# Gate logits in six tiles of 128 tokens, finished inside the down product, with x sums, GpSimd's weight work and the first Sinkhorn hops at other places

## The chip, the cores and the metric

The kernel runs on one NeuronCore of a Trainium2 chip. The metric is device time in microseconds of one execution; lower is better. PE is TensorE, DVE is VectorE, ACT is ScalarE, POOL is GpSimd, SP is the queue that issues the transfers.

## What is computed

Sliding-window attention (4 batches, 8 heads, 576 positions, 64 wide, window 64) feeds a dense layer with an ELU, and that feeds a layer of eight experts whose output is weighted by a gate. The gate is what the change touches.

```python
def _moe_ref(x, w_in, w_out):                 # x 2304 x 512, d_ff 2048
    h = x @ w_in
    g = np.where(h > 0.0, h, alpha * (np.exp(np.minimum(h, 0.0)) - 1.0))
    return (g @ w_out)

def _moe2_ref(x, w_gate, w1, w2):             # 8 experts, F 1024
    logits = x @ w_gate
    logits = logits - logits.max()
    P = np.exp(logits)
    for _ in range(8):
        P /= P.sum(1, keepdims=True) + 1e-09
        P /= P.sum(0, keepdims=True) + 1e-09
        P *= N / E
    for e in range(E):
        h = np.maximum(x @ w1[e], 0.0)
        ye = h @ w2[e]
        out += P[:, e:e + 1] * ye
```

## The kernel before

After the attention the program goes through 60 rounds: 20 groups of 512 hidden columns (4 of the dense layer, 16 of the experts), each for 3 chunks of 768 tokens. The block products are done with seven products in place of eight (a Strassen form), so a round has seven up products (`ps<-xs,w1t`) and seven down products (`ps<-ss,w2t`). Each product is 12 matmuls of 128 x 384: three for each of four operand pairs, since every operand is a high and a low part (`hi`, `lo`). The kernel's loop goes by windows w: window w does the up steps of round w and the down steps of round w-1 in turn, up 0, down 0, up 1, down 1, to step 6. I write up (w,s) for the up product of step s in window w, and down (w,s) for the down product that follows it in the same window.

All five engines run hand-written orders and are joined by counting semaphores; there is no scheduler. In each window ACT copies products out of PSUM (`snap_*`, L710) and makes the high parts (`hi`, L763); DVE adds products (`add_c`, L970), adds the down products to the sum `yacc` (`add_y`, L1044), makes low parts (`lo`, L942), the activation (`act_f`, L1017; `relu` on ACT, L788, for some rounds) and the Strassen sums s1 to s4 (L949 to L965); POOL splits weights (`weight_sum_*`, `weight_lo`, L542 to L565). A semaphore counts each: `c_done` up products, `d_done` down products, `c_read` the `add_c`, `s_lo_done` the `lo`, `y_read` and `y_copied` the `add_y` of a step. `wait_f(engine, r, 4)` waits until the fourth activation of round r is there; up (w,1) needs it of round w-1.

Windows 11 to 13 (`GATE_WINDOW` to before `MAX_WINDOW`) have extra work. The dense layer's result of chunk c is ready in `yacc` then, and DVE and ACT turn it into the experts' operand: four sums of quarters (`x_sum`, L984 to L998, places in the table `XSUMS`) and seven high and low parts (`x_hi` L683, `x_lo` L905, places in `XPREP`), which up products of window 12 and later read directly. In the same windows PE makes the gate's logits in `hop`, which `product` calls in the middle of an up product, after 7 of its 12 matmuls:

- steps 1, 2 and 3: two token tiles each, a matmul for every quarter of the 512 columns of x, the four into four groups of 32 partitions (L1339);
- a step later ACT has put these parts into `logit_parts` (`move_parts`, L718), and PE adds the four groups up with the constant `adder` (L1331), transposed, into free columns of the up product's banks; ACT (L721) or DVE (L1091) moves eight logits for each token to `gate`;
- the last two of the eight tiles of 96 tokens are done at step 1 the other way round, with `yacc` as the weights and eight moving columns (L1348).

From window 14 come the eight Sinkhorn steps: DVE normalises rows and sums columns over tiles (`rows_then_parts`), PE sums over partitions (a hop, L1361), DVE normalises columns (`columns`). The list `SINK_HOPS` says at which up product each hop stands. After the eighth the table is turned and stored, and window 18 is the first that uses it.

Of the kernel before, what the change touches and what calls it, by code (L numbers as in the profile page):

```python
# [12 lines left out]
P = 128  # L13
# [14 lines left out]
def build_program(nc, q, k, v, w_in, w_out, w_gate, w1, w2, out):  # L28
# [39 lines left out]
    TT = 96  # L68
# [14 lines left out]
    for w, cc in [(1, 2)] + [(GATE_WINDOW + c, CHUNKS + c) for c in range(CHUNKS)]:  # L83
# [5 lines left out]
        XSUMS[0 if cc < CHUNKS else w][0 if cc < CHUNKS else 3] = [(cc, 0), (cc, 1)]  # L89
# [34 lines left out]
    SINK_HOPS = [(MAX_WINDOW, 3), (MAX_WINDOW, 5)]  # L124
# [4 lines left out]
    with ExitStack() as ctx:  # L129
# [25 lines left out]
        p_turned = logit_parts[0:TT]  # L155
# [82 lines left out]
        def hop_spare(w, step):  # L238
            return spare(w, step, 0, HT + TT + 4 * step, HT + TT + 4 * step + E)[0:TT, :]

        def c_spare(r, step, a, b):
            s = (r + step) % 2
            return ps[:, 2 * s:2 * s + 2, a:b]

# [77 lines left out]
        stored = sem("stored")  # L322

# [77 lines left out]
        def _(sp):  # L401
# [70 lines left out]
            for w in range(ROUNDS):  # L472
                g, c = divmod(w, CHUNKS)
                e, half = divmod(g - FF_GROUPS, HALVES)
                for step in range(STEPS):
# [8 lines left out]
                    if w == SCALE_WINDOW - 1 and step == 1:  # L484
                        for i in range(2):
                            sp.wait_ge(p_placed, 1)
                            sp.dma_start(p_store[i * TT:(i + 1) * TT, :], p_turned[:, i, :]).then_inc(p_stored, 16)
# [24 lines left out]
        def _(pool):  # L512
# [88 lines left out]
            for w in range(ROUNDS):  # L601
# [18 lines left out]
                if w >= 1:  # L620
                    pool.wait_ge(s_lo_done, STEPS * (w - 1) + STEPS)
# [25 lines left out]
        def _(act):  # L647
# [64 lines left out]
            def tiles(w, first):  # L712

                t = (w - GATE_WINDOW) * CHUNK_TILES + first
                return gate[:, :, t:t + 2].rearrange("p e t -> p t e")

            def move_parts(w, step):
                nc.scalar.activation(logit_parts[:], c_spare(w, step, HT, HT + TT), ACT.Copy).then_inc(parts_placed, 1)  # L718

            def move_logits(w, step, first, at):  # L720
                nc.scalar.activation(tiles(w, first), c_spare(w, step, HT + at, HT + at + E)[0:TT], ACT.Copy) \  # L721
                    .then_inc(logits_moved, 1)

            def gate_work(w, step):
# [3 lines left out]
                if step == 1:  # L728
                    move_logits(w, step, CHUNK_TILES - 2, TT + E)
                else:  # L730
                    move_logits(w, step, 2 * (step - 2), TT)
                move_parts(w, step)
# [75 lines left out]
            for w in range(ROUNDS + 1):  # L808
# [49 lines left out]
                gate_work(w, 1)  # L858
# [3 lines left out]
                gate_work(w, 2)  # L862
# [6 lines left out]
                gate_work(w, 3)  # L869
# [20 lines left out]
        def _(dve):  # L890
# [177 lines left out]
            def columns(k):  # L1068
# [6 lines left out]
                elif step == 5:  # L1075
                    dve.wait_ge(c_done, STEPS * w + step + 1)
                nc.vector.tensor_scalar(col_norm[0:TT], hop_spare(w, step), EPS, None, ALU.add).then_inc(col_read, 1)
# [10 lines left out]
            def gate_work(w, at):  # L1088
                if at == 4 and GATE_WINDOW <= w < MAX_WINDOW:
                    t = (w - GATE_WINDOW) * CHUNK_TILES + 4  # L1090
                    nc.vector.tensor_copy(gate[:, :, t:t + 2].rearrange("p e t -> p t e"),  # L1091
                                          c_spare(w, 4, HT + TT + E, HT + TT + 2 * E)[0:TT]).then_inc(logits_placed, 1)
                if w == MAX_WINDOW - 1 and at == 4:
                    dve.wait_ge(logits_placed, CHUNKS)
                    dve.wait_ge(logits_moved, 3 * CHUNKS)
                    nc.vector.tensor_reduce(token_max[0:TT], gate[:], AX.XY, ALU.max).then_inc(token_maxed, 1)
                if w == MAX_WINDOW - 1 and at == 5:
                    dve.wait_ge(max_turned, 1)
                    dve.wait_ge(c_done, STEPS * w + 6)
                    nc.vector.tensor_reduce(all_max[:], spare(w, 5, 0, HT, HT + TT)[0:1, :], AX.X, ALU.max,  # L1100
                                            negate=True).then_inc(all_maxed, 1)
                if w == MAX_WINDOW and at == 0:
# [3 lines left out]
                    nc.vector.tensor_copy(gate_shift[0:TT], spare(w, 0, 0, HT + TT, HT + TT + 1)[0:TT, :]) \  # L1106
# [11 lines left out]
                if (w, at) == P_HOP:  # L1118
# [3 lines left out]
                    nc.vector.tensor_copy(p_turned, c_spare(w, at, HT, HT + TT)[0:TT]).then_inc(p_placed, 1)  # L1122

            def x_piece(w, at):
                for cc, i in XSUMS[w][at]:
                    x_sum(cc, i)
# [302 lines left out]
```

## Time and profile before

| | |
|---|---|
| time, median of 3 runs | 1929.63 us (1926.22 to 1929.71) |
| the profiled execution | 1927.98 us, of which its span 1926.1 us |
| busy share of the span | PE 98%, DVE 79%, ACT 44%, POOL 34% |
| chain that ended last | PE 90%, DVE 5% |
| three kinds of large matmul of up and down, 1680 each | 10080, mean 336 to 339 ns, overlapped in pairs |

A busy PE is not a PE at its peak, since matmuls overlap. A timeline's first column is the start in us from the span's start, the second the length; the distance from one start to the next is what an instruction costs on PE. In brackets stands how long the engine idled before it and what released it.

### The profile page before, as it was taken

What the parts mean: (1) busy time and instruction counts of PE and PEld (TensorE: products, weight loads), DVE (VectorE), ACT (ScalarE), POOL (GpSimd) and SP (SyncE); (2) the same over time, 40 slices, a digit from 0 to 9 for tenths busy, and PEclk for the clock granted to TensorE, in tenths of its full rate; (3) what the DMA queues carried; (4) which work ended last, traced back from release to release, by engine and by line L of the source; (5) the groups of instructions that cost most, each with busy time, mean ns of one, the idle gap of its engine ahead of it and who ended that gap; (6) DMA issues with size and microseconds to landing.
All of it is one profiled execution on the core that took longest, in us unless ns stands there. A gap on an engine that the chain in (4) does not pass through costs nothing.

```text
span 1926.1 us, 31391 instructions
## 1 busy us (share of the span) xinstructions
PE 1883.2 (98%) x11676; PEld 1847.0 (96%) x11676; DVE 1526.8 (79%) x1840; ACT 853.1 (44%) x1419; POOL 651.9 (34%) x512
## 2 busy tenths in 40 slices
PE   8889999999999999999999999999999999999998
PEld 6669999998889999999999999999999999999998
DVE  6987878777889888787787787787787787877877
ACT  7767656555556443343333342332433332433422
POOL 5643332332232434332423324233323233233220
PEclk9999999999999999999999999999999999999999
DMA  9974766663357666666566666666666666666654
GB/s 250 278 283 143 250 215 206 216 207 134 152 194 243 237 223 215 222 225 235 200 241 213 217 213 226 212 216 227 218 231 207 229 221 211 219 227 210 212 187 148
DMA packets 96710, 414.75 MB, mean 215 GB/s; under 512 B 9776, under 2 KB 10800, under 8 KB 96560
## 3 DMA queue, kind: packets, MB, share of 16 engines
q1 hardware_dynamic: 96560, 412.74, 63.0%
q8 instruction: 95, 1.56, 0.3%
q14 instruction: 55, 0.45, 0.1%
HBM read 374.88 MB, written 37.82 MB: 214 GB/s over the span
## 4 chain that ended last, share of the span: by engine, by line
PE 90%; DVE 5%; issue 2%; ACT 1%; POOL 1%; DMA 1%; DVEq 0%; SPq 0%; ACTq 0%; POOLq 0%
PE ps L1269 29%; PE ps L1264 29%; PE ps L1271 29%; PE ps L1228 1%; PE ps L1254 1%; DMA scratch<-v_dram 1%; PE ps L1244 1%; DVE hb L1017 1%; DVE xs L905 0%; DVE hb L970 0%; DVE ss L942 0%; DVE scratch L919 0%; ACT pb L775 0%; POOL scratch L536 0%; DVE yacc L1044 0%
## 5 line engine op out<-in xcount | busy, mean ns | idle before, releaser
L763 ACT ACTIVATE ss<-hb 128x768 fp32r<-128x768 f32 x420 | 347.8, 843 | 602.1 <-DVE hb L1024 281.4
L1264 PE MATMUL ps<-xs,w1t 128*128 128x384 f32 x1680 | 569.0, 339 | 8.9 <-DVE hb L1017 4.1
L1269 PE MATMUL ps<-xs,w1t 128*128 128x384 f32 x1680 | 569.5, 339 | 0.0
L1264 PE MATMUL ps<-ss,w2t 128*128 128x384 f32 x1680 | 564.5, 336 | 2.5 <-DVE yacc L1044 2.5
L1271 PE MATMUL ps<-ss,w2t 128*128 128x384 f32 x1680 | 566.1, 337 | 0.0
L1271 PE MATMUL ps<-xs,w1t 128*128 128x384 f32 x1680 | 566.0, 337 | 0.0
L1269 PE MATMUL ps<-ss,w2t 128*128 128x384 f32 x1680 | 563.9, 336 | 0.0
L1044 DVE TENSOR_TENSOR yacc<-ps,yacc 128x768 f32<-128x768 f32 x396 | 377.9, 954 | 176.8 <-PE ps L1271 171.7
L942 DVE TENSOR_TENSOR ss<-hb,ss 128x768 fp32r<-128x768 f32 x420 | 400.0, 956 | 21.8 <-ACT ss L763 11.5
L565 POOL TENSOR_TENSOR w1t<-wraw,w1t 128x512 fp32r<-128x512 f32 x140 | 187.3, 1350 | 511.9 <-DVE ss L942 327.4
L565 POOL TENSOR_TENSOR w2t<-wraw,w2t 128x512 fp32r<-128x512 f32 x140 | 183.7, 1330 | 427.0 <-DVE hb L965 229.0
L1264 PEld LDWEIGHTS ps<-xs,w1t 128*128 128x128 f32 x1680 | 315.8, 188 | 11.1 <-issue 6.7
L1264 PEld LDWEIGHTS ps<-ss,w2t 128*128 128x128 f32 x1680 | 316.8, 189 | 3.7 <-DVE ss L942 2.5
L1269 PEld LDWEIGHTS ps<-xs,w1t 128*128 128x128 f32 x1680 | 316.8, 189 | 1.1 <-issue 0.2
L1271 PEld LDWEIGHTS ps<-xs,w1t 128*128 128x128 f32 x1680 | 316.6, 188 | 0.0
L1271 PEld LDWEIGHTS ps<-ss,w2t 128*128 128x128 f32 x1680 | 316.5, 188 | 0.0
L1269 PEld LDWEIGHTS ps<-ss,w2t 128*128 128x128 f32 x1680 | 316.5, 188 | 0.0
L970 DVE TENSOR_TENSOR hb<-ps,hb 128x768 f32<-128x768 f32 x180 | 172.1, 956 | 138.6 <-PE ps L1271 138.1
L710 ACT ACTIVATE hb<-ps 128x768 f32<-128x768 f32 x180 | 145.2, 807 | 156.7 <-PE ps L1271 155.7
L1024 DVE SCALAR_TENSOR_TENSOR hb<-hb,pb 128x768 f32<-128x768 f32 x126 | 130.6, 1036 | 2.9
L660 ACT ACTIVATE w2t<-wraw 128x512 fp32r<-128x512 f32 x140 | 87.1, 622 | 89.5 <-PE ps L1271 89.5
L542 POOL TENSOR_TENSOR wraw<-wraw 128x512 f32<-128x512 f32 x40 | 53.1, 1328 | 194.0 <-DVE hb L965 194.0
(100 smaller groups left out, 1342.6 us busy)
## 6 DMA issues: line engine op xcount, KB each, us to landing
xs<-x_store SPq DMA_DIRECT2D x388, 768.0 KB, 4.3
wraw<-moe_w_dram SPq DMA_DIRECT2D x32, 1024.0 KB, 7.0
x_store<-xs SPq DMA_DIRECT2D x32, 768.0 KB, 4.1
pb<-p_store SPq DMA_DIRECT2D x24, 384.0 KB, 4.0
x_store<-w2t SPq DMA_DIRECT2D x10, 768.0 KB, 3.9
scratch<-q_dram SPq DMA_DIRECT2D x16, 288.0 KB, 4.9
scratch<-k_dram SPq DMA_DIRECT2D x16, 288.0 KB, 7.5
scratch<-v_dram SPq DMA_DIRECT2D x16, 288.0 KB, 7.8
```

Source lines behind the costliest of these rows:

```text
L542: nc.gpsimd.tensor_tensor(wtmp[i][:, 0], w_quarter(i, 0, 1), w_quarter(i, 0, 0), ALU.subtract) \
L565: nc.gpsimd.tensor_tensor(pair2(wt[i][:, step, 1, :]), w_operand(i, step), pair2(wt[i][:, step, 0, :].bitcast(F32)), ALU.subtract) \
L660: nc.scalar.activation(pair2(wt[i][:, step, 0, :]), w_operand(i, step), ACT.Copy) \
L710: nc.scalar.activation(pair2(hq(r, quarter)), c_banks(r, step), ACT.Copy).then_inc(c_snap, 1)
L763: nc.scalar.activation(ss[:, step, 0, :], hq(r, HOME[step]), ACT.Copy).then_inc(s_hi_done, 1)
L942: nc.vector.tensor_tensor(ss[:, step, 1, :], hq(r, HOME[step]), ss[:, step, 0, :].bitcast(F32), ALU.subtract).then_inc(s_lo_done, 1)
L970: nc.vector.tensor_tensor(pair2(hq(r, quarter)), c_banks(r, step), pair2(hq(r, quarter)), ALU.add) \
L1024: nc.vector.scalar_tensor_tensor(h, src, 0.0, weight, ALU.max, ALU.mult).then_inc(f_done, 1)
L1044: nc.vector.tensor_tensor(acc, d_banks(r, step), acc, ALU.add).then_inc(y_read, 1)
L1264: nc.tensor.matmul(bank, w_parts[:, step, 0, cols], hi, start=step in FRESH and kt == 0, stop=False, skip_group_check=True)
L1269: nc.tensor.matmul(bank, w_parts[:, step, 0, cols], lo, start=False, stop=False, skip_group_check=True)
L1271: last = nc.tensor.matmul(bank, w_parts[:, step, 1, cols], hi, start=False, stop=kt == 1, skip_group_check=True)
```

## The change

The tiles are 128 tokens, so six instead of eight for each chunk and 18 in all. All six are made by quarters (steps 1, 2 and 3, tiles 4-5, 0-1 and 2-3), and the `yacc`-as-weights form is gone. The adding up stands one product later, in the middle of down step 2, 3 or 4, in the free columns of the down product's bank (`d_spare`). `move_parts` at steps 2 and 3 now waits for that step's down product too. All logits of a chunk are moved by two copies instead of four. Hop 1 no longer waits for the last add to `yacc` (step 6 of round w-2), only for step 5; hop 2 waits for step 6. On DVE the first two x sums go from place 3 to place 2 of the window, ahead of `add_y` of step 3. POOL's third batch of weight work in windows 11 to 13 waits for `add_c` of step 4 instead of a low part that is long there. The first two Sinkhorn hops go from window 14's steps 3 and 5 to steps 4 and 6, DVE's parts of them with them. The turn of the maxima goes into down step 5.

```diff
-    TT = 96
+    TT = P
-        XSUMS[0 if cc < CHUNKS else w][0 if cc < CHUNKS else 3] = [(cc, 0), (cc, 1)]
+        XSUMS[0 if cc < CHUNKS else w][0 if cc < CHUNKS else 2] = [(cc, 0), (cc, 1)]
-    SINK_HOPS = [(MAX_WINDOW, 3), (MAX_WINDOW, 5)]
+    SINK_HOPS = [(MAX_WINDOW, 4), (MAX_WINDOW, 6)]
...
+        GATE_TILES = {1: 4, 2: 0, 3: 2}
...
-                if w >= 1:
+                if GATE_WINDOW <= w < MAX_WINDOW:
+                    pool.wait_ge(c_read, 3 * w + 2)
+                elif w >= 1:
                     pool.wait_ge(s_lo_done, STEPS * (w - 1) + STEPS)
...
             def move_parts(w, step):
-                nc.scalar.activation(logit_parts[:], c_spare(w, step, HT, HT + TT), ACT.Copy).then_inc(parts_placed, 1)
-            def move_logits(w, step, first, at):
-                nc.scalar.activation(tiles(w, first), c_spare(w, step, HT + at, HT + at + E)[0:TT], ACT.Copy) \
-                    .then_inc(logits_moved, 1)
-            def gate_work(w, step):
                 if not GATE_WINDOW <= w < MAX_WINDOW:
                     return
                 act.wait_ge(c_done, STEPS * w + step + 1)
+                if step >= 2:
+                    act.wait_ge(d_done, STEPS * (w - 1) + step + 1)
+                nc.scalar.activation(logit_parts[:], c_spare(w, step, HT, HT + TT), ACT.Copy).then_inc(parts_placed, 1)
...
             def gate_work(w, at):
+                if at == 3 and GATE_WINDOW <= w < MAX_WINDOW - 1:
+                    dve.wait_ge(d_done, STEPS * (w - 1) + 4)
+                    nc.vector.tensor_copy(logits_of(w - GATE_WINDOW, 0, 2), summed(w, 3, 0, 2)).then_inc(logits_placed, 1)
                 if at == 4 and GATE_WINDOW <= w < MAX_WINDOW:
+                    dve.wait_ge(d_done, STEPS * (w - 1) + 5)
+                    nc.vector.tensor_copy(logits_of(w - GATE_WINDOW, 2, CHUNK_TILES), summed(w, 4, 2, CHUNK_TILES)) \
+                        .then_inc(logits_placed, 1)
...
                 x_piece(w, 2)
+                gate_work(w, 3)
                 if down:
                     add_y(before, 3)
...
                 x_piece(w, 3)
-                gate_work(w, 3)
...
-                product(d_banks(r, step), step, w2t, step, ss, d_done)
+                product(d_banks(r, step), step, w2t, step, ss, d_done, between=lambda: down_hop(r + 1, step))
...
                     if step == 1:
-                        wait_y(pe, FF_ROUNDS - CHUNKS + c1, 6)
+                        wait_y(pe, FF_ROUNDS - CHUNKS + c1, 5)
+                    if step == 2:
+                        wait_y(pe, FF_ROUNDS - CHUNKS + c1, 6)
-                    if step >= 2:
-                        pe.wait_ge(parts_placed, 3 * c1 + step - 1)
...
-                    if step == 1:
-                        for j in range(2):
-                            first = c1 * CT + (CHUNK_TILES - 2 + j) * TT
-                            at = HT + TT + E
-                            for kt in range(KT):
-                                nc.tensor.matmul(spare(w, step, j, at, at + E)[0:TT, :], yacc[:, kt, first:first + TT],
-                                                 wg[:, kt, 0:E], start=False, stop=kt == KT - 1, skip_group_check=True)
...
+            def down_hop(w, step):
+                if GATE_WINDOW <= w < MAX_WINDOW and step - 1 in GATE_TILES:
+                    pe.wait_ge(parts_placed, 3 * (w - GATE_WINDOW) + step - 1)
+                    for j in range(2):
+                        t = GATE_TILES[step - 1] + j
+                        nc.tensor.matmul(d_spare(w - 1, step, 0, E * t, E * (t + 1)), logit_parts[:, j, :], adder[:],
+                                         start=False, stop=True, skip_group_check=True)
```

PE's order, in window 11 before, the middle of up step 2 (`xs,w1t` is an up product):

```order
L1264 MATMUL ps<-xs,w1t 128x384
L1331 MATMUL ps<-adder,logit_parts 96x8 x2
L1339 MATMUL ps<-yacc,wg 32x96 x8
L1269 MATMUL ps<-xs,w1t 128x384
L1271 MATMUL ps<-xs,w1t 128x384
```

and now, the same place and on into down step 2 (`ss,w2t`):

```order
L1292 MATMUL ps<-xs,w1t 128x384
L1362 MATMUL ps<-yacc,wg 32x128 x8
L1297 MATMUL ps<-xs,w1t 128x384
...
L1299 MATMUL ps<-ss,w2t 128x384
L1292 MATMUL ps<-ss,w2t 128x384
L1389 MATMUL ps<-adder,logit_parts 128x8 x2
L1297 MATMUL ps<-ss,w2t 128x384
```

The adding up moved from the head of the hop in the up product to the middle of the next product, 12 large matmuls later.

DVE's order in window 12 before, from the low part of step 6 (`ss<-hb,ss`); `yacc<-ps,yacc` is `add_y`, `yacc<-yacc` and `pb<-yacc` are the first two x sums, `hb<-ps,hb` is `add_c` of step 4:

```order
L942 TENSOR_TENSOR ss<-hb,ss 128x768
L905 TENSOR_TENSOR xs<-yacc,xs 128x768
L1044 TENSOR_TENSOR yacc<-ps,yacc 128x2x384
L984 TENSOR_TENSOR yacc<-yacc 128x2x384
L990 TENSOR_TENSOR pb<-yacc 128x768
L905 TENSOR_TENSOR xs<-yacc,xs 128x768 x2
L970 TENSOR_TENSOR hb<-ps,hb 128x768
L1091 COPY gate<-ps 96x2x8
```

and now:

```order
L956 TENSOR_TENSOR ss<-hb,ss 128x768
L919 TENSOR_TENSOR xs<-yacc,xs 128x768
L998 TENSOR_TENSOR yacc<-yacc 128x2x384
L1004 TENSOR_TENSOR pb<-yacc 128x768
L1108 COPY gate<-ps 128x2x8
L1058 TENSOR_TENSOR yacc<-ps,yacc 128x2x384
L919 TENSOR_TENSOR xs<-yacc,xs 128x768 x2
L984 TENSOR_TENSOR hb<-ps,hb 128x768
L1111 COPY gate<-ps 128x4x8
```

The two x sums stand ahead of `add_y` of step 3, with a first small copy of logits between them.

POOL's order in window 11 before, with the semaphores that each instruction waits for; `w1t` is weight_lo, `wraw` a weight sum:

```order
L565 TENSOR_TENSOR w1t<-wraw,w1t 128x512 [waits w_hi_done0,s_lo_done]
L548 TENSOR_TENSOR wraw<-wraw 128x2x256 [waits w_added1]
L565 TENSOR_TENSOR w1t<-wraw,w1t 128x512 [waits w_hi_done0,s_lo_done]
L565 TENSOR_TENSOR w1t<-wraw,w1t 128x512 [waits w_hi_done0]
L552 TENSOR_TENSOR wraw<-wraw 128x512
```

and now:

```order
L580 TENSOR_TENSOR w1t<-wraw,w1t 128x512 [waits w_hi_done0,s_lo_done]
L563 TENSOR_TENSOR wraw<-wraw 128x2x256 [waits w_added1]
L580 TENSOR_TENSOR w1t<-wraw,w1t 128x512 [waits w_hi_done0,c_read]
L580 TENSOR_TENSOR w1t<-wraw,w1t 128x512 [waits w_hi_done0]
L567 TENSOR_TENSOR wraw<-wraw 128x512
```

The last three of these now stand behind DVE's `add_c` of step 4.

## Rows read from the trace of the kernel before

**Rows 1.** Busy time of the engines by stretches: us, then PE, PEld, DVE, ACT, POOL, clock

```profile
437.30:585.00 147.70, 136.97 (x907) 131.28 (x906) 119.02 (x140) 82.40 (x128) 46.05 (x31) 0.97 0.44 157
585.00:1926.00 1341.00, 1334.58 (x7665) 1333.10 (x7664) 1066.08 (x1181) 490.58 (x676) 424.34 (x317) 1.00 0.63 217
```

**Rows 2.** Who waited for whom, 440 to 660 us: total us, times, longest

```profile
PE ps L1361 <- DVE col_part L1066: 3.5, 2, 2.0
...
PE ps L1331 <- ACT logit_parts L718: 2.9, 3, 1.9
...
PE ps L1339 <- DVE yacc L1044: 1.9, 1, 1.9
PE ps L1264 <- DVE hb L1017: 1.5, 1, 1.5
...
PE ps L1264 <- DVE xs L905: 0.5, 1, 0.5
```

**Rows 3.** Timeline of PE in window 11

```profile
443.33 1.52 PE L1348 MATMUL ps<-wg,yacc 128*96 128x8 f32 x16
444.71 0.43 PE L1269 MATMUL ps<-xs,w1t 128*128 128x384 f32 x1
...
451.07 0.51 PE L1331 MATMUL ps<-adder,logit_parts 128*96 128x8 f32 x4 [1.90 <-ACT logit_parts L718]
...
456.62 0.54 PE L1339 MATMUL ps<-yacc,wg 128*32 128x96 f32 x16
457.08 0.44 PE L1269 MATMUL ps<-xs,w1t 128*128 128x384 f32 x1
...
461.37 0.42 PE L1331 MATMUL ps<-adder,logit_parts 128*96 128x8 f32 x4
461.65 0.42 PE L1269 MATMUL ps<-xs,w1t 128*128 128x384 f32 x1
```

**Rows 4.** Timeline of PE in window 12

```profile
482.26 0.87 PE L1339 MATMUL ps<-yacc,wg 128*32 128x96 f32 x16 [1.93 <-DVE yacc L1044]
483.06 2.73 PE L1348 MATMUL ps<-wg,yacc 128*96 128x8 f32 x16
485.64 0.67 PE L1269 MATMUL ps<-xs,w1t 128*128 128x384 f32 x1
...
488.58 0.33 PE L1269 MATMUL ps<-ss,w2t 128*128 128x384 f32 x1
```

**Rows 5.** Timeline of PE in window 14

```profile
576.71 0.34 PE L1361 MATMUL ps<-col_part,ones 96*96 96x8 f32 x2 [1.96 <-DVE col_part L1066]
...
580.62 0.34 PE L1269 MATMUL ps<-ss,w2t 128*128 128x384 f32 x1
```

**Rows 6.** Timeline of DVE in window 11

```profile
460.34 0.96 DVE L1044 TENSOR_TENSOR yacc<-ps,yacc 128x768 f32<-128x768 f32 x1 [3.28 <-PE ps L1271]
461.21 1.79 DVE L984 TENSOR_TENSOR yacc<-yacc 128x768 f32<-128x768 f32 x1
463.04 1.93 DVE L990 TENSOR_TENSOR pb<-yacc 128x768 f32<-128x768 f32 x1
...
466.71 0.94 DVE L1044 TENSOR_TENSOR yacc<-ps,yacc 128x768 f32<-128x768 f32 x1
```

**Rows 7.** Timeline of POOL in window 11

```profile
462.12 2.03 POOL L552 TENSOR_TENSOR wraw<-wraw 128x512 f32<-128x512 f32 x1
```

**Rows 8.** Timeline of ACT in window 11

```profile
450.71 0.32 ACT L718 ACTIVATE logit_parts<-ps 128x192 f32<-128x192 f32 x1
...
458.34 0.81 ACT L710 ACTIVATE hb<-ps 128x768 f32<-128x768 f32 x1 [3.51 <-PE ps L1271]
```

**Rows 9.** Timeline of DVE in window 14

```profile
570.95 1.13 DVE L905 TENSOR_TENSOR xs<-yacc,xs 128x768 fp32r<-128x768 f32 x1 [3.34 <-ACT xs L683]
572.00 0.15 DVE L1077 TENSOR_SCALAR col_norm<-ps 96x8 f32<-96x8 f32 x1
...
576.57 0.94 DVE L970 TENSOR_TENSOR hb<-ps,hb 128x768 f32<-128x768 f32 x1
```

More of the change, by code:

```diff
@@ L238, in hop_spare @@
         def hop_spare(w, step):
-            return spare(w, step, 0, HT + TT + 4 * step, HT + TT + 4 * step + E)[0:TT, :]
+            return spare(w, step, 0, HT + E * step, HT + E * (step + 1))[0:TT, :]
         def c_spare(r, step, a, b):
@@ L322, in build_program, with logits_of, summed @@
         stored = sem("stored")
+        GATE_TILES = {1: 4, 2: 0, 3: 2}
+        def logits_of(c, first, last):
+            t = c * CHUNK_TILES
+            return gate[:, :, t + first:t + last].rearrange("p e t -> p t e")
+        def summed(w, step, first, last):
+            return d_spare(w - 1, step, 0, E * first, E * last).rearrange("p (t e) -> p t e", e=E)
         def unit(n, lag):
@@ L1324, in hop @@
                             pe.wait_ge(adder_made, 1)
+                        wait_y(pe, FF_ROUNDS - CHUNKS + c1, 5)
+                    if step == 2:
                         wait_y(pe, FF_ROUNDS - CHUNKS + c1, 6)
-                    if step >= 2:
-                        pe.wait_ge(parts_placed, 3 * c1 + step - 1)
-                        at = HT + TT + (E if step == 4 else 0)
-                        for j in range(2):
-                            nc.tensor.matmul(spare(w, step, j, at, at + E)[0:TT, :], logit_parts[:, j, :], adder[:],
-                                             start=False, stop=True, skip_group_check=True)
@@ L1333, in hop @@
-                    if step <= 3:
-                        for j in range(2):
-                            first = c1 * CT + (2 * (step - 1) + j) * TT
-                            for kt in range(KT):
-                                quarter = slice(kt * P // KT, (kt + 1) * P // KT)
-                                nc.tensor.matmul(spare(w, step, j, HT, HT + TT)[quarter, :], wg[:, kt, :],
-                                                 yacc[:, kt, first:first + TT], start=False, stop=True,
-                                                 skip_group_check=True)
@@ L1400, in _ @@
                     if w >= 1:
+                        down_hop_read(w, step)
                         down_step(w - 1, step)
```

92 lines of the change are left out of this document (55 added, 37 removed).

## The prediction

> **What bounds the kernel now.** I read busy time by stretches first. From 585 us on PE is busy for 1334.58 of 1341.00 us; in the gate's stretch, 437.3 to 585 us, for 136.97 of 147.70 us, at a granted clock of 0.97, with DVE busy for 119.02 us, 81% [rows 1]. So PE bounds the kernel, and this stretch has 10.7 us in which it stands still. The change touches windows 11 to 14 (and the first Sinkhorn steps), all in it.
>
> Next, who PE waits for there: the parts of the logits from ACT 2.9 us in three waits; `yacc` from DVE 1.9; DVE's last activation of window 11 1.5; an x low part 0.5; the column parts of the first two Sinkhorn hops 3.5 [rows 2]. Together 10.3.
>
> Last, PE's timeline. The L1348 block (tiles 6 and 7) lasts from 443.33 to 444.71, 1.38 us. A block of quarters lasts 0.46 (456.62 to 457.08), an adder pair 0.28 (461.37 to 461.65). Between 457.08 and 461.37 stand 24 large matmuls, 4.29 us; with some 0.1 lost at each hop that is the usual pace of 0.173 us for one, 2.08 for a product [rows 3]. In window 12 two waits come close together, and behind them everything is slower: the L1348 block takes 2.58 us (483.06 to 485.64), and nine starts take 2.94 (485.64 to 488.58) where 1.56 is usual [rows 4]. The same stands behind the second Sinkhorn wait: 13 starts in 3.91 us (576.71 to 580.62) instead of 2.25 [rows 5]. The granted clock below 1 for the stretch [rows 1] says that PE ran at the lower of its two levels there. These half-clock stretches cost 1.20 + 1.38 + 1.66 = 4.2 us.
>
> **The change part by part.**
>
> *Tiles 6 and 7 go:* three blocks at 1.38 = 4.1 us (what the second took above that is in the 4.2).
>
> *128 columns instead of 96 in nine blocks of quarters.* No row has a block of 128. Below: nothing, if issue sets the 0.46. Above: in proportion, 0.46 x 32/96 = 0.15 each, 1.4 in all. A quarter-block has some start-up in it, so I take 0.11 each: 1.0 us lost.
>
> *Adder pairs on their own.* Their number stays nine, but six no longer share a hop with quarters. A pair alone takes 0.28 where the next matmul would start after 0.17 [rows 3], and leaving a hop costs that 0.1 once more: 0.7 lost, 0 to 1.3.
>
> *The wait for the parts (2.9).* In window 11 PE would have been ready at 451.07 - 1.90 = 449.17. Now it needs the parts after a block of quarters and 12 large matmuls: 449.17 + 0.6 + 2.08 = 451.8. ACT has them at 450.71 + 0.32 = 451.0 [rows 3, 8]. Slack 0.8; the other two waits were shorter. Gone: 2.9. ACT's new wait for the down product (steps 2 and 3) is for a product that ends 2.08 later than the up product it waited for. Behind it in ACT's queue stand `copy_y`, which waits for that down product anyway, an `x_hi`, a `weight_hi` and `snap_p7`, whose own up product ends another 2.08 later. Parts of steps 2 and 3 are needed a whole up product and a half later. Cost 0, because ACT sits idle there: 3.51 us before the copy at 458.34 [rows 8]; without that cover each `x_hi` would come up to 2.1 late.
>
> *The wait for `yacc` in window 12 (1.9).* Hop 1 needs only step 5, added in the window before. Step 6 is now wanted at hop 2, over 4 us later. Gone: 1.9. With it goes the half-clock stretch in window 12, since of the two waits ahead of it one goes and the other shrinks: 1.20 + 1.38 = 2.6.
>
> *x sums earlier, POOL later (the waits 1.5 and 0.5).* In window 11 DVE idles 3.28 us up to `add_y` of step 3 at 460.34, then does the two sums from 461.21 to 464.9. They may start when the third up product is done, which ACT's copy shows at 458.34 [rows 6, 8], 2.9 earlier. How much of it arrives? `add_y` of step 4 stood at 466.71, while its down product ends 17 matmuls behind the hop at 461.65, at 464.6 [rows 3, 6]. So the train behind it can move up by 2.1 at most, against a PE wait of 1.5. The sums themselves took 1.79 and 1.93 us beside POOL's 2.03 at 462.12, where DVE's `add_y` of the same size takes 0.94 [rows 6, 7]: 1.8 us of contention, which the POOL wait is to take off. It does not vanish. POOL's five or six instructions now begin at `add_c` of step 4 and lie beside activations, x low parts and s3. Move 2.1 up against a wait of 1.5 and 0.6 is to spare; one or two contended DVE instructions in that train at 0.8 each (1.79 against 0.96) eat it: the activation is ready 0.6 before PE wants it, or up to 1.0 after. I take both waits as gone, 2.0, and what may come back is in the 2.0 lost below. The added logit copy hides in DVE's idle time.
>
> The Trainium skill speaks against this part: in "SBUF — State Buffer", section "SBUF: two separate sides", the port pair that VectorE and GpSimd share is an exclusive lock, held for a whole instruction, against VectorE instructions with two SBUF inputs. The rows above agree: the sums (two SBUF inputs) pay, `add_y` (one from PSUM) does not. By that rule contention only moves with POOL's work, to instructions nearer to what PE waits for; this is the first rival below.
>
> *First Sinkhorn hops a product and a half or more later (3.5, and the half-clock stretch 1.66).* The first hop goes from up step 3 to 4, 4.2 us later, against a wait under 2: gone. The second goes from 5 to 6, again 4.2 against 1.96. Its DVE work, `columns` and `rows_then_parts`, took from 572.00 to 576.57, 4.57 us, ahead of `add_c` of step 4 [rows 9]; now it stands behind it. Tables are 144 instead of 192 columns, about 0.3 less a step. But PE gains 5 us in this window and DVE does not lose work. Taking PE's waits out of the window leaves it about 29.6 us for its 14 products and hops; DVE had about 34 us up to the low part that down (15,1) needs, of which 3.34 is one idle stretch [rows 9], so some 30 us of work. So DVE becomes the later one: I put 1.5 us on it, at up (14,4), up (14,6) or down (15,1). Window 12 gets 0.5 the same way, since DVE loses there the time in which it used to wait for PE. 2.0 lost, 0 to 5.
>
> *The turn of P* stores 144 rows of 128 instead of 192 of 96: far from PE's path, cost 0; uncovered it would be under a few tenths.
>
> **Sum.** Gained 4.1 + 10.3 + 4.2 = 18.6; lost 1.0 + 0.7 + 2.0 = 3.7; net 14.9 us. The profiled execution took 1927.98 (span 1926.1 and 1.9 around it), so 1913.1. The median of the runs is 1.65 higher, which gives 1914.7; the runs spread over 3.5. I take 1913.5.
>
> **Rivals.**
>
> *DVE is late again (0.16).* Contention lands on the activations, the waits 1.5 and 0.5 come back, window 14 keeps 3.5 as waits for low parts and its half-clock 1.7 too: 18.6 - 7.2 - 1.7 = 9.7 gained, about 1918.5. For: DVE 81% busy [rows 1] and the lock. Against: the idle 3.28 and 3.34 us that the new order fills or frees.
>
> *The clock still falls (0.08).* Waits shrink but several short stops lie close together, and PE runs at half clock in two stretches: 14.9 - 4.2 = 10.7 gained, 1917.5. For: nothing in the rows says how little idling is enough. Against: no large stop is left.
>
> *The waits only change their name (0.05).* The parts and `yacc` waits turn into waits at the down steps: only 4.1 + 1 - 1.7 = 3.4 gained, 1925.
>
> *Slower (0.04).* ACT is the place: its wait for the down product delays `x_hi` and `snap_p7` by up to 2.1 us at steps 2 and 3 of three windows, six times, 12.5, and each window then gets a half-clock stretch like window 12's 2.6, 7.8: 20.3 against 14.9, so 5.4 slower, 1933. It decides from the point where more than four of the six reach PE with their half-clock stretches. Against: ACT's 3.51 idle at this place [rows 8].
>
> The forecast itself, with a gain of 12 to 19, has 0.67.
>
> **How the numbers follow.** About 0.2% (4 us) is what a measurement of this kernel can tell. The low end: all of 18.6 less 0.7 from the fastest shown run, 1926.22, gives 1908.3. The high end takes in the first two rivals: 1921. Left out: the last two and some of the first, together under 0.2; the forecast's own range is 1909 to 1917. Faster: 0.67 + 0.16 + 0.08 + a part of the third, 0.91; same: 0.05; slower: 0.04.
>
> **What would show it.** In the changed profile: no L1348 blocks, nine blocks of quarters of 0.5 to 0.62; no PE wait for `logit_parts` or `yacc`; granted clock 1.00 from 437 us to window 15; the hop waits for `col_part` gone, DVE without an idle stretch over 3 us beside it in window 14; POOL's batch behind `add_c` of step 4, x sums near 0.95 each and DVE instructions late in the window at 1.3 to 1.7. The prediction is wrong if PE waits over 3 us in the stretch, most likely for `hb L1017`, `xs` or `ss` from DVE, or if starts 0.32 apart show up again.

## The result, and the profile after

| | before | changed |
|---|---|---|
| median (all runs) | 1929.49 us (1926.22 to 1930.55, 10 runs) | 1921.64 us (1919.51 to 1924.41, 10 runs) |
| span of the profiled execution | 1926.1 us | 1919.8 us |

The ratio is 0.9959, with a 95% interval of 0.995 to 0.9967: 7.9 us faster, where 16 had been forecast (1929.49 against 1913.5). The time lies 0.6 us above the stated range.

Busy time of the changed kernel by stretches, with the columns of [rows 1]; the gate's stretch now ends at 577 us:

```profile
437.30:577.00 139.70, 136.56 (x882) 130.21 (x882) 125.83 (x151) 86.23 (x126) 46.37 (x31) 0.99 0.48 177
577.00:1919.00 1342.00, 1337.18 (x7643) 1335.95 (x7641) 1059.78 (x1174) 486.94 (x671) 423.39 (x317) 1.00 0.64 216
```

PE idles 3.1 us in the gate's stretch where it idled 10.7, and DVE is busy for 90% of it. The second row tells what I had not looked for: 7643 matmuls in 1342 us, where [rows 1] has 7665 in 1341. In a stretch that the change hardly touches, PE never idles for long in either kernel, and yet it gets through less.

Who waited for whom in the changed kernel, 437 to 650 us (total us, times, longest):

```profile
ACT logit_parts L738 <- PE ps L1299: 8.7, 6, 1.8
...
PE ps L1292 <- issue: 2.8, 1, 2.8
...
PE ps L1292 <- DVE yacc L1058: 0.3, 1, 0.3
```

Of the five waits of PE in [rows 2] none is left. Two others stand there: 0.3 for `yacc`, and a single one of 2.8 that the view puts down to "issue". PE's timeline of windows 11 and 12:

```profile
443.18 0.65 PE L1362 MATMUL ps<-yacc,wg 128*32 128x128 f32 x16
443.75 0.44 PE L1297 MATMUL ps<-xs,w1t 128*128 128x384 f32 x1
...
450.94 0.51 PE L1389 MATMUL ps<-adder,logit_parts 128*128 128x8 f32 x4
451.30 0.42 PE L1297 MATMUL ps<-ss,w2t 128*128 128x384 f32 x1
...
478.42 0.41 PE L1292 MATMUL ps<-ss,w2t 128*128 128x384 f32 x1 [0.34 <-DVE yacc L1058]
478.67 0.34 PE L1297 MATMUL ps<-ss,w2t 128*128 128x384 f32 x1
```

A block of quarters takes 0.57 (0.46 in [rows 3]), an adder pair 0.36 (0.28), and the adding up waits for nothing. Of window 14:

```profile
564.50 0.34 PE L1299 MATMUL ps<-ss,w2t 128*128 128x384 f32 x1
567.64 0.49 PE L1292 MATMUL ps<-xs,w1t 128*128 128x384 f32 x1 [2.80 <-issue]
567.92 0.52 PE L1297 MATMUL ps<-xs,w1t 128*128 128x384 f32 x1
568.24 0.52 PE L1299 MATMUL ps<-xs,w1t 128*128 128x384 f32 x1
...
569.84 0.43 PE L1372 MATMUL ps<-col_part,ones 128*128 128x8 f32 x2
570.12 0.67 PE L1297 MATMUL ps<-xs,w1t 128*128 128x384 f32 x1
...
571.23 0.35 PE L1297 MATMUL ps<-xs,w1t 128*128 128x384 f32 x1
```

Up (14,6) starts 2.80 us late, and its starts are then 0.32 apart up to 571.23: the granted clock from 567.83 to 571.24 is 0.50, the lower of TensorE's two levels (1.2 of 2.4 GHz). Starts 0.32 apart were one of the signs that the prediction named for being wrong. Those ten large matmuls and the hop take 3.59 us, where 10 x 0.174 + 0.28 = 2.02 is usual: 1.6 more. DVE ahead of that start:

```profile
559.02 0.94 DVE L984 TENSOR_TENSOR hb<-ps,hb 128x768 f32<-128x768 f32 x1
559.89 0.15 DVE L1094 TENSOR_SCALAR col_norm<-ps 128x8 f32<-128x8 f32 x1
560.07 0.20 DVE L1096 RECIPROCAL col_norm<-col_norm 128x8 f32<-128x8 f32 x1
560.31 1.22 DVE L1098 TENSOR_SCALAR col_norm<-col_norm 128x8 f32<-128x8 f32 x1
561.57 1.35 DVE L1101 TENSOR_TENSOR gate<-gate,col_norm 128x144 f32<-128x144 f32 x1
...
563.39 0.71 DVE L1073 TENSOR_SCALAR row_norm<-row_norm 128x18 f32<-128x18 f32 x1
...
564.44 1.03 DVE L1077 TENSOR_TENSOR gate<-gate,row_norm 128x144 f32<-128x144 f32 x1
565.51 0.30 DVE L1080 TENSOR_REDUCE col_part<-gate 128x8 f32<-128x144 f32 x1
565.73 0.95 DVE L1058 TENSOR_TENSOR yacc<-ps,yacc 128x768 f32<-128x768 f32 x1
566.59 0.95 DVE L919 TENSOR_TENSOR xs<-yacc,xs 128x768 fp32r<-128x768 f32 x1
```

and POOL beside it:

```profile
558.23 3.27 POOL L580 TENSOR_TENSOR w1t<-wraw,w1t 128x512 fp32r<-128x512 f32 x2
561.47 1.28 POOL L567 TENSOR_TENSOR wraw<-wraw 128x512 f32<-128x512 f32 x1
562.71 2.59 POOL L580 TENSOR_TENSOR w1t<-wraw,w1t 128x512 fp32r<-128x512 f32 x2
```

By DVE's order the releaser is the x low part that ends at 567.5 (L919); "issue" only says that the view found no event. Ahead of it in DVE's queue stand the nine Sinkhorn instructions, from 559.89 to 565.73, 5.84 us.

### The profile page after: what moved, and what is told of

The parts are those of the page before. It is cut to its first block, busy times and chain, and to the rows that moved or that the text cites. A ratio compares the mean times of both kernels' runs of the same rounds, so it can differ in the third digit from the quotient of the medians.

```text
span 1919.8 us, 31295 instructions
## 1 busy us (share of the span) xinstructions
PE 1886.1 (98%) x11628; PEld 1849.9 (96%) x11628; DVE 1526.9 (80%) x1842; ACT 853.3 (44%) x1411; POOL 651.0 (34%) x512
## 4 chain that ended last, share of the span: by engine, by line
PE 92%; DVE 3%; issue 2%; DMA 2%; ACT 1%; POOL 1%; SPq 0%; DVEq 0%; POOLq 0%; ACTq 0%
PE ps L1297 29%; PE ps L1292 29%; PE ps L1299 29%; PE ps L1256 2%; DMA x_store<-xs 1%; PE ps L1282 1%; PE ps L1272 1%; DVE hb L1031 0%; DVE scratch L933 0%; DVE scratch L927 0%; PE ps L1249 0%; DVE w2t L919 0%; DVE ss L956 0%; DVE hb L984 0%; PE ps L1362 0%
```

## Two theories, and where the lost time stands

I split both traces at one matmul block that both have, the first block of quarters (442.86 before, 443.18 changed), and at the turn of P in window 17. Before:

```profile
646.77 0.50 PE L1366 MATMUL ps<-ident,gate 96*96 96x96 f32 x4
```

Changed:

```profile
635.09 0.60 PE L1377 MATMUL ps<-ident,gate 128*72 128x128 f32 x4
```

Between the two points 203.91 us became 191.91: 12.0 gained, not far from the forecast 14.9. Behind them 1926.1 - 646.77 = 1279.33 us became 1919.8 - 635.09 = 1284.71: 5.4 lost, where PE's matmuls are the same but for the turn itself. And 0.3 was lost ahead of the first point. 12.0 - 5.4 - 0.3 = 6.3, the difference of the spans.

**The pace theory.** Three tables change size for 128-token tiles: per partition `gate` 768 to 576 bytes, `row_norm` 96 to 72, `logit_parts` 768 to 1024. The sum is 40 bytes more; with each table rounded up to a multiple of 32 bytes `row_norm` takes 96 in either case, which makes it 64. So `ss`, the down products' moving operand, starts at byte 161280 of each partition instead of 161216, and `hb` also 64 further on; `yacc`, `xs`, `w1t` and `w2t` stay. Something in that place sets the pace of the matmuls.

**The rival.** The later work (windows 12 on) runs against changed neighbours: POOL's batch, DVE's order, the clock. The loss would then not follow a table's place.

The steady stretch tells the pace best, since PE is never idle in it. Before, 700 to 1700 us:

```profile
700.00:1700.00 1000.00, 1000.00 (x5744) 1000.00 (x5743) 792.25 (x859) 359.67 (x498) 329.04 (x250) 1.00 0.65 220
```

Changed:

```profile
700.00:1700.00 1000.00, 1000.00 (x5716) 1000.00 (x5715) 787.33 (x852) 358.34 (x496) 328.81 (x250) 1.00 0.65 219
```

1000 us hold 5744 matmuls before and 5716 in the changed kernel, 174.1 and 174.9 ns each, at a granted clock of 1.00 in both. That is 4.9 us over this stretch, nearly all of the 5.4 lost behind the second point.

## The experiments on the pace

All ratios below are against the kernel before on the same chip, where its median was 1928.2 to 1929.1 us. So kernels of different experiments are best compared by their ratios. Where an expectation says A and B, these are the theories that it states itself.

**The changed kernel with `ss` at its old byte.** Two small tables go behind `hb`:

```diff
-        col_part = sb("col_part", [P, E])
-        col_norm = sb("col_norm", [P, E])
         logit_parts = sb("logit_parts", [P, 2, TT])
...
         hb = sb("hb", [P, 2, 4, QN])
+        col_part = sb("col_part", [P, E])
+        col_norm = sb("col_norm", [P, E])
```

> The changed kernel with col_part and col_norm allocated behind hb, so that ss and hb start at the same SBUF bytes as in the kernel before (161216 and 204224, 64 bytes lower); no instruction differs. Theory A (the missing gain is pace, and the pace hangs on where ss and hb lie): a down product in windows 1 to 10 and 18 to 60 goes back from 2.11 to 2.08 us, an up product from 2.09 to 2.10, about 0.018 us a pair over some 410 pairs, 7 us less: 1914 us, ratio to before 0.992. Theory B (the pace comes from the instruction stream or from the run, not from the place): no change, 1921.6 us, ratio 0.996, down products stay at 2.11.

Measured: 1914.8 us, 0.9927 (0.9913 to 0.9941); the changed kernel had 0.9959. Its steady stretch is back at the old count:

```profile
700.00:1700.00 1000.00, 1000.00 (x5744) 1000.00 (x5743) 790.66 (x857) 360.99 (x499) 329.00 (x249) 1.00 0.65 220
```

and so are the distances between the split points:

```profile
441.97 0.65 PE L1362 MATMUL ps<-yacc,wg 128*32 128x128 f32 x16
...
633.27 0.60 PE L1377 MATMUL ps<-ident,gate 128*72 128x128 f32 x4
```

191.30 us, 12.6 gained; 1911.8 - 633.27 = 1278.53 behind it. No order and no wait was edited. By the ratios 0.32% hung on 64 bytes, some 6 us (6.8 by the medians, 1921.64 - 1914.8).

**The kernel before with 64 bytes in front of `ss` and `hb`.**

```diff
         warm = sb("warm", [P, 1])
+        pad = sb("pad", [P, 16])
```

> The kernel before with one unused tensor of 64 bytes ahead of scratch, ss and hb, so that these lie where the changed kernel has them; no instruction differs. Theory A: down products go from 2.08 to 2.11 us and the time up by 7 us, to 1936.5 us, ratio 1.0035 to 1.004. Theory B: ratio 1.000, within 0.05%.

Measured: 1934.85 us, 1.003 (1.0018 to 1.0041), and 5716 matmuls in the steady stretch. The loss appears in a kernel without a line of the change. The pace theory stands, its rival falls.

**Only `hb` 64 bytes further on.**

```diff
         ss = sb("ss", [P, STEPS, 2, QN], F32R)
+        pad = sb("pad", [P, 16])
         hb = sb("hb", [P, 2, 4, QN])
```

> The kernel before with 64 unused bytes between ss and hb: ss stays, only hb starts 64 bytes later; no instruction differs. Theory A (the down product's pace hangs on the place of ss, which it reads as moving operand; hb is touched by DVE and ACT only): products stay at 2.10 and 2.08 us, ratio 1.000 within 0.1%. Theory B (it is hb's place, through DVE's and ACT's accesses): ratio 1.003, as with both moved, down products 2.11.

Measured: 1930.11 us, 0.9999 (0.999 to 1.0008), 5744 matmuls. `hb`, which PE does not read, has no part in it. It is `ss`.

**`ss` and `hb` 128, 192 and 256 bytes further on**: the pad of the second experiment with 32, 48 and 64 words.

> The kernel before with 128 unused bytes ahead of scratch, ss and hb. Theory A (what counts is the start modulo 128 bytes): products back at 2.10 and 2.08 us, ratio 1.000. Theory B (a larger period, or any move): down products stay at 2.11 or take a third value, ratio 1.003 or more.

> The kernel before with 192 unused bytes ahead of scratch, ss and hb (ss at byte 161408). Theory A (the pace repeats with 128 bytes, on top of a drift): like 64 bytes, down products 2.11 us, ratio 1.001 to 1.003. Theory B (each place has its own pace): a value apart from those of 0, 64 and 128.

> The kernel before with 256 unused bytes ahead of scratch, ss and hb. Theory A (a period of 256 bytes): 5744 matmuls in the stretch, ratio 1.000. Theory B (longer or no period): another count, the ratio apart from 1 by 0.1% or more.

**All tables 64 bytes further on**, so that the distances between `yacc`, `xs`, the weights and `ss` stay:

```diff
+        pad = sb("pad", [P, 16])
         yacc = sb("yacc", [P, KT, N])
```

> The kernel before with 64 unused bytes ahead of all its tensors: xs, w1t, w2t, ss and hb all start 64 bytes later, their distances stay. Theory A (the distance of ss to the other operands counts): the count of matmuls in 700 to 1700 us stays at 5744, ratio 1.000. Theory B (the absolute place of ss counts): 5716 as with ss alone moved, ratio 1.003. A third count would say that xs or the weights have a pace of their own as well.

The columns "up" and "down" are the mean time from a product's first start to the next product's, over the 237 to 240 plain products of each kind in the 1000 us.

| kernel before, with | matmuls in 1000 us | ns each | up, down us | median us | ratio (95%) |
|---|---|---|---|---|---|
| nothing | 5744 | 174.1 | 2.105, 2.075 | 1929.5 | 1 |
| `ss`, `hb` +64 | 5716 | 174.9 | 2.083, 2.117 | 1934.85 | 1.003 (1.0018 to 1.0041) |
| `ss`, `hb` +128 | 5762 | 173.6 | 2.091, 2.076 | 1924.79 | 0.998 (0.9972 to 0.9989) |
| `ss`, `hb` +192 | 5771 | 173.3 | 2.080, 2.080 | 1923.69 | 0.997 (0.996 to 0.998) |
| `ss`, `hb` +256 | 5744 | 174.1 | 2.105, 2.075 | 1928.32 | 1.0000 (0.9991 to 1.0009) |
| all +64 | 5744 | 174.1 | 2.105, 2.075 | 1930.01 | 1.0006 (0.9997 to 1.0015) |

At 128 bytes neither theory was right: the one asked for the old count, the other for a loss, and the count rose. At 192 and 256 bytes the theories B and A held, and with all tables moved A.

The last row but one shows the old pace again after 256 bytes, the last one that moving all together changes nothing. So it is the distance of `ss` to tables ahead of it, and among the places tried it repeats after 256 bytes. (`hb` moved with `ss` in these; alone it was tried at 64 bytes only.) The row that stands for the best place, of the kernel with +192:

```profile
700.00:1700.00 1000.00, 1000.00 (x5771) 1000.00 (x5771) 798.08 (x864) 360.92 (x500) 331.39 (x251) 1.00 0.65 222
```

The mean DVE, ACT and POOL instruction takes the same to within 1%; only PE's starts lie closer. With +192 each of the 12 matmuls of either product starts 173.2 to 173.4 ns after the one before, by the means over the stretch. In the other places some of the 12 are late: up to 185.0 ns in the first seven of an up product at the old place, up to 181.6 in the down product with +64. The up products read `xs` and `w1t`, which did not move, and yet gain or lose with the place of `ss`; so the effect is not confined to the products that read `ss`. Which of the tables ahead it is, whether it is PE's reading or another engine's access that meets PE's, and why, was not tried and stays open.

## The experiments on the gate's stretch

**POOL's third batch back at the low part**, nothing else, on the changed kernel:

```diff
-                if GATE_WINDOW <= w < MAX_WINDOW:
-                    pool.wait_ge(c_read, 3 * w + 2)
-                elif w >= 1:
+                if w >= 1:
                     pool.wait_ge(s_lo_done, STEPS * (w - 1) + STEPS)
```

> The changed kernel with POOL's third batch in windows 11 to 13 waiting for the low part again instead of add_c of step 4. Theory A (the later POOL batch frees the x sums, and what it costs at the window's end is hidden): the x sums take 1.8 and 1.9 us again, DVE's last activation of window 11 is about 1 us later and PE waits up to 1 us for it: 1 to 2 us slower than the changed kernel, 1923. Theory B (contention only moves): same time within 0.5 us, 1921.6, ratio 0.996.

Measured: 1919.28 us, 0.9954 (0.9942 to 0.9967), no different from the changed kernel's 0.9959. But the trace has a wait that the later batch takes away:

```profile
499.84 0.45 PE L1289 MATMUL ps<-xs,w1t 128*128 128x384 f32 x1 [1.41 <-DVE xs L916]
```

and the 0.3 for `yacc` is gone in return. The 1.1 us between them are too few to be seen in the times. This trace also shows something of window 14. Up (14,6) waits as long as in the changed kernel, but the granted clock (third figure from the end of the second row, which is busy time by stretches) stays at 1.00 behind it:

```profile
566.85 0.41 PE L1289 MATMUL ps<-xs,w1t 128*128 128x384 f32 x1 [2.81 <-issue]
...
566.85:570.26 3.41, 3.41 (x20) 3.41 (x21) 3.25 (x4) 2.61 (x4) 0.00 (x0) 1.00 0.48 72
```

A wait of 2.80 us was followed by the lower level in one execution, and one of 2.81 was not in another. The 1.6 us of half clock are thus not a fixed price of the wait.

**The first two Sinkhorn hops back at steps 3 and 5:**

```diff
-    SINK_HOPS = [(MAX_WINDOW, 4), (MAX_WINDOW, 6)]
+    SINK_HOPS = [(MAX_WINDOW, 3), (MAX_WINDOW, 5)]
```

> The changed kernel with the first two Sinkhorn hops back at steps 3 and 5 of window 14. Theory A (moving the hops is worth 3.5 us of waits and 1.7 us at half clock, of which up (14,6) gives back 3.0 and 1.5): about 1 to 2 us slower than the changed kernel, 1923. Theory B (in window 14 DVE decides, wherever the hops are): within 0.5 us of it, with PE waiting at the hops instead of at up (14,6).

Measured: 1920.54 us, 0.9954 (0.9942 to 0.9967). PE waits twice and not once in window 14:

```profile
555.41 0.39 PE L1372 MATMUL ps<-col_part,ones 128*128 128x8 f32 x2 [1.17 <-DVE col_part L1080]
...
564.78 0.41 PE L1292 MATMUL ps<-xs,w1t 128*128 128x384 f32 x1 [1.68 <-issue]
```

1.17 + 1.68 = 2.85 against 2.80, and the clock does not fall behind them in this execution. Moving the hops took the wait away from the hop and gave it to the next product: DVE was late by its work, not by where the hops stood.

**The x sums back at place 3**, on the first experiment's kernel:

```diff
-        XSUMS[0 if cc < CHUNKS else w][0 if cc < CHUNKS else 2] = [(cc, 0), (cc, 1)]
+        XSUMS[0 if cc < CHUNKS else w][0 if cc < CHUNKS else 3] = [(cc, 0), (cc, 1)]
```

> The changed kernel with ss and hb at their old place and the first two x sums back at place 3, behind add_y of step 3. Theory A (the earlier x sums are what removes PE's waits for the activation of window 11 and for x low parts in window 12): waits of 0.5 to 2 us come back at up (12,1), up (12,5) or up (12,6), 1 to 3 us slower than e1, 1917. Theory B (the waits are gone because the waits ahead of them and the half clock are gone): within 0.5 us of e1, 1914.8.

Measured: 1915.41 us, 0.9929 (0.9917 to 0.9942), against 0.9927. The wait of window 12 comes back in the trace, 1.34 us for DVE's last activation at 475.06 (1.5 in [rows 2]), with 0.23 for a low part; the time can't tell these from nothing. Between the split points it can be told: 635.00 - 441.95 = 193.05 us against 191.30, 1.8 more, with one half-clock stretch in either trace, in window 14.

**Hop 1 waits for step 6 of `yacc` again**, on the same kernel:

```diff
-                        wait_y(pe, FF_ROUNDS - CHUNKS + c1, 5)
+                        wait_y(pe, FF_ROUNDS - CHUNKS + c1, 6)
```

> e1 with hop 1 waiting for the add of step 6 of the round before, as in the kernel before. Theory A (this wait is a term of its own): PE waits about 2 us at hop 1 of window 12, and with it parts of the half-clock stretch come back, 2 to 4 us more than e1, 1917 to 1919. Theory B (it was only long because DVE was late): the wait is under 1 us, 1915.

Measured: 1917.03 us, 0.9939 (0.9925 to 0.9953), 2.2 us slower than without it by the medians, though the intervals overlap.

```profile
477.94 0.65 PE L1362 MATMUL ps<-yacc,wg 128*32 128x128 f32 x16 [1.91 <-DVE yacc L1058]
```

The wait is that of [rows 4], 1.93, and here too the lower clock level follows it, for 3.41 us:

```profile
478.49:481.90 3.41, 3.41 (x15) 3.39 (x12) 3.31 (x5) 2.09 (x4) 1.29 (x1) 0.50 0.12 43
```

11 large matmuls from 478.51 to 482.07 take 3.56 us instead of 1.91. Between the split points stand 636.64 - 442.85 = 193.79 us against 191.30, 2.5 more. So one wait alone was enough for a half-clock stretch, shorter than the 5.5 us behind two waits in [rows 4].

**In window 14 the x low part ahead of the Sinkhorn work**, on the first experiment's kernel:

```diff
-                gate_work(w, 4)
+                if w != MAX_WINDOW:
+                    gate_work(w, 4)
...
                 x_piece(w, 4)
+                if w == MAX_WINDOW:
+                    gate_work(w, 4)
```

> The changed kernel with ss and hb at their old place (as in e1) and, in window 14, DVE's first column and second row step behind add_y of step 4 and the x low part that up (14,6) waits for. Theory A (the 3 us stop at up (14,6) is DVE order: 5.8 us of Sinkhorn work ahead of that low part): the stop at up (14,6) shrinks to 1 to 1.5 us at the hop and the stretch at half clock behind it goes: 3 us less than e1, 1912 us. Theory B (DVE is simply full in window 14): the stop moves to the hop or to window 15 in full length, 1914.8 us.

Measured: 1912.56 us, 0.9917 (0.9904 to 0.9929), 2.2 below 1914.8.

```profile
567.64 0.39 PE L1375 MATMUL ps<-col_part,ones 128*128 128x8 f32 x2 [2.31 <-DVE col_part L1080]
567.89 0.42 PE L1300 MATMUL ps<-xs,w1t 128*128 128x384 f32 x1
568.15 0.33 PE L1302 MATMUL ps<-xs,w1t 128*128 128x384 f32 x1
```

Up (14,6) starts on time and PE waits at its hop instead, 2.31 us. Behind the first of these, starts are 0.17 apart. In this trace it is 0.5 us less of waiting and no half clock, where the first experiment's had some 1.5: 632.03 - 442.72 = 189.31 us between the split points, 2.0 less. Only the 0.5 is the order's for certain, as the last experiment below shows.

**And POOL's batch of window 14 behind the Sinkhorn work as well:**

```diff
+                elif w == MAX_WINDOW:
+                    pool.wait_ge(col_parted, 2)
```

> e7 with one more wait: in window 14 POOL's third batch starts behind the column parts of the second Sinkhorn step. Theory A (the DVE chain ahead of the second hop is stretched by POOL: 4.7 us in e7 where the same nine instructions take 2.5 alone): the chain takes 2.5 to 3 us, PE's wait of 2.3 us at the hop in up (14,6) falls under 0.5, nothing new appears in window 15: 2 us less than e7, 1910.5 us. Theory B (window 14 is full either way): POOL's late batch makes PE wait in window 15 for weights, 1912.5 us or more.

Measured: 1914.9 us, 0.9929 (0.9917 to 0.9942), no gain, the median 2.3 higher. DVE's timeline shows why:

```profile
561.10 0.17 DVE L1100 TENSOR_SCALAR col_norm<-col_norm 128x8 f32<-128x8 f32 x1
561.30 0.31 DVE L1103 TENSOR_TENSOR gate<-gate,col_norm 128x144 f32<-128x144 f32 x1
...
562.94 0.30 DVE L1082 TENSOR_REDUCE col_part<-gate 128x8 f32<-128x144 f32 x1
...
565.09 1.60 DVE L965 TENSOR_TENSOR hb<-hb 128x768 f32<-128x768 f32 x1
566.73 1.93 DVE L969 TENSOR_TENSOR hb<-hb 128x768 f32<-128x768 f32 x1
568.58 2.04 DVE L958 TENSOR_TENSOR ss<-hb,ss 128x768 fp32r<-128x768 f32 x1
```

Without POOL beside them the nine instructions take 2.5 us (560.66 to 563.16) instead of 5.84 (4.69 in the kernel with the low part first), and PE's hop waits for nothing. But POOL then runs from 563.33 on beside the sums and a low part, which take 1.60 to 2.04 where 0.96 is usual, and PE waits in window 15: 1.17 for `col_norm` and 1.55 for `col_part`, with slow starts behind. Contention moved; it was not removed.

**The best orders with a better place.** The last kernel with `ss` 128 bytes further on, and the one with the low part first, without POOL's new wait, 192 further on (a pad of 48 words in the same place):

```diff
         warm = sb("warm", [P, 1])
+        pad = sb("pad", [P, 32])
```

> e10 with ss and hb 128 bytes higher (ss at byte 161344, as in e6). Theory A (the pace with ss there is a property of the place and adds to any schedule): 0.2% less than e10, 1907 us, ratio 0.989. Theory B (it needs the old schedule): same as e10.

> e7 (changed schedule, window 14's low part first) with ss and hb 192 bytes above the old place. Theory A (place and schedule add): e7's 0.9917 times e12's 0.997, 1907 us, and below the 0.9901 of e9. Theory B (the place's gain depends on the schedule): 1909 or more.

Measured: 1909.35 us, 0.9901 (0.9887 to 0.9914), and 1906.68 us (1906.61 to 1906.88), 0.9883 (0.987 to 0.9897). The second beats both kernels, the changed one by 15 us, and has 5771 matmuls in the steady stretch. The gain of the place adds to that of the order: 0.9917 to 0.9883 is 0.34%, and 192 bytes on the kernel before are worth 0.30% (0.997).

The second has the order of the kernel with the low part first, and the same wait at the same hop. Yet here the lower level follows:

```profile
566.55 0.39 PE L1376 MATMUL ps<-col_part,ones 128*128 128x8 f32 x2 [2.31 <-DVE col_part L1081]
...
567.52:570.93 3.41, 3.41 (x13) 3.40 (x12) 3.26 (x4) 3.32 (x5) 0.00 (x0) 0.50 0.84 234
```

## Why the prediction was wrong

**The step that failed** is "The change touches windows 11 to 14 (and the first Sinkhorn steps), all in it". The sum carries the stretch's 14.9 us over to the whole kernel, and so puts a change of pace in the other 1280 us at nothing, without a reason. The prediction looks at the tables' new sizes only for the instructions that use them ("Tables are 144 instead of 192 columns", and the turn of P), and gives their place no price. The place cost some 6 us in this kernel (0.9959 against 0.9927) and as much in the kernel before (1.003). With `ss` back, the time is 1914.8, 1.3 above the forecast and inside its own range; some of that closeness is luck, since the stretch gained 2.3 less than the sum had it, and 1.7 us that no experiment explains were gained outside it (below). None of the rivals had this mechanism; that the result stands near the 1918.5 and 1925 of two of them says nothing for those.

**The term that was mis-sized** is "2.0 lost", DVE late in windows 12 and 14. Window 12 has 0.34 (0.5 was taken). Window 14 has 2.80 + 1.6 of half clock = 4.4 (1.5 was taken). The working had the place right, up (14,6), and DVE's 30 us of work against 29.6 for PE; it had the Sinkhorn instructions at about their old cost of 4.57 [rows 9]. In that cost POOL already had a part (one on `gate` took 1.40 beside it), and the new order laid more of POOL's batch over them, which in window 14 still starts at the old low part. Beside POOL four of the nine take 1.22, 1.35, 0.71 and 1.03 where 0.17, 0.31, 0.18 and 0.31 are enough, which the kernel with POOL's batch later shows; together 3.3 us more, the whole difference between 2.5 and 5.84. "DVE is late again" (0.16) was in this window the better description, though the waits 1.5 and 0.5 of windows 11 and 12 that it wanted back are gone.

**Point by point, what held.** Quarters: +0.11 a block, measured 0.57 against 0.46. Adder pair alone: 0.36 where I had taken 0.28. The parts' wait is gone; ACT idles for 8.7 us in six waits for the product, and PE never waits for ACT in this stretch. The `yacc` wait at hop 1 and the half-clock stretch of window 12 are gone. That the stretch went with the wait fits the experiment on hop 1, where both came back. That removing waits buys a full clock in general does not hold: in the seven traces of the kernel before, with and without a pad, the first wait is the same, 1.9 us at the hop of window 11; 3.41 us at 0.50 follow it in five, and not in the other two (no pad, and `ss` and `hb` +64). And the granted clock of the kernel before went from 0.992 to 0.995 over the ten executions beside the first experiment (1932.01 and 1926.19 us). In window 11 the sums are earlier and partly cheaper:

```profile
455.33 1.14 DVE L998 TENSOR_TENSOR yacc<-yacc 128x768 f32<-128x768 f32 x1 [1.04 <-PE ps L1299]
456.50 1.93 DVE L1004 TENSOR_TENSOR pb<-yacc 128x768 f32<-128x768 f32 x1
...
464.48 2.04 DVE L919 TENSOR_TENSOR xs<-yacc,xs 128x768 fp32r<-128x768 f32 x1
```

The first at 1.14 instead of 1.79, the second still 1.93, and an x low part that now takes 2.04. The rule from the Trainium skill ("SBUF — State Buffer", section "SBUF: two separate sides") that the prediction weighed, an exclusive lock for a whole instruction, agrees with that and with the two POOL experiments: delaying POOL only chooses which DVE instructions are slow. All of the slow ones read SBUF twice but L1098 and L1073, each with a single SBUF table as its input; for such the same section names another case, a VectorE instruction in a two-port performance mode, and whether these run in one no row here shows. Shown is that slow DVE instructions follow POOL's; the lock itself is not.

**In sum.** At the old place the stretch gained 12.6 where 14.9 was forecast: 4.4 - 1.5 = 2.9 more lost in window 14 (2.86 of wait and some 1.5 of half clock in that trace), 0.2 less in window 12, and 0.4 gained for a wait of 0.43 in the kernel before that the 10.3 left out (the view puts it down to "issue"). The kernel as changed then lost 0.6 more there, and 5.4 + 0.3 outside. A further 1.7 us that the first experiment's profiled execution gained outside the stretch (0.9 ahead, 0.8 behind) is below what the runs scatter by. Part of the stretch's gain is of the same uncertain kind, since a half-clock stretch of 3.41 us costs some 1.6 and is there in one execution and not in another.

**Which parts were worth it.** By the times, neither POOL's later batch, nor the moved x sums, nor the moved hops makes a measurable difference by itself, though the first two each take a wait of over 1 us out of the trace. The waits around them are of one late engine, and what one edit frees, DVE's next late instruction takes. The split of `yacc`'s wait is worth some 2 us by the medians and 2.5 between the split points, though the intervals of the times overlap. What is left of 12.6 is with the two tiles fewer, the adding up one product later and the half-clock stretches; these were not tried apart.

## What to carry to other kernels

When a change resizes any table, compare where the operands of the steady loop start before and after, and count matmuls in a stretch that the change does not touch: here a pace that differed by 0.5% cost as much as several of the removed waits together. A gain that is foreseen for one stretch should be measured in that stretch, between two matmul blocks that both kernels have, before any story is told about the whole. Read the granted clock of that stretch too: a half-clock stretch that is missing after the change may be missing by chance. And when an engine is 80 to 90% busy beside the bound, moving its deadline or its neighbour moves the wait; price the train of instructions at what they cost beside the other engine, not alone.

## What the runs showed of the hardware

- The pace of back-to-back 128 x 384 matmuls, at a granted clock of 1.00, depends on where the moving operand of one of the two loops starts, relative to tables ahead of it: 174.9, 174.1, 173.6 and 173.3 ns each at four places 64 bytes apart, and the same again after 256. The matmuls of the other loop, whose operands stayed, change with it (2.105 and 2.083 us for an up product). The 0.9% between the ends is 11 us of this kernel (1934.85 against 1923.69).
- A half-clock stretch does not go by the length of the wait ahead of it. PE at full clock waited 2.80 us and 3.41 us of the lower level followed; it waited 2.81 in the kernel with POOL's batch early, and none followed. It waited 2.31 us at the same hop in two kernels of one order; the lower level followed in the one with `ss` 192 bytes on, and not in the other. Waits of 1.9 us had it behind them (the kernel with hop 1 waiting for step 6, and window 11 of the kernel before with +128) or not (window 11 of the kernel before as it is). What decides stays open.
- Beside POOL, a DVE instruction on 8 columns took 1.22 us instead of 0.17, and one on 144 columns 1.35 instead of 0.31. They ended at 561.53 and 562.92, and POOL's instructions beside them changed at 561.47 and 562.71: by these two, what is lost goes by POOL's instruction, not by the length of DVE's own.
